# Attention with top-k and two gated products in one kernel: the first token tile normalised while it is turned, its x gathered pair by pair, the second tile scaled sooner

## The reference

```python
# q, k, v: 2 x 8 heads x 576 x 64, f32
scores = scale * q @ k.T
kth = the 32nd largest of a row
scores = where(scores >= kth, scores, -1e9)
attn = exp(scores - max); attn /= (sum(attn) + 1e-9)
x = attn @ v                     # laid as 1152 tokens x 512
x = ((x @ w_a) * (x @ w_b)) @ w_out      # w_a, w_b: 512 x 1536
p = probs / sum(probs)
out = sum over 4 experts e of p[:, e] * (relu(x @ w1[e]) @ w2[e])
```

## Time and profile before

| | us |
|---|---|
| median of 3 runs | 809.16 (808.32 to 809.25) |
| the profiled execution | 809.39 |
| its span | 807.6 |
| PE busy | 774.5 (96%) |
| DVE busy | 570.8 (71%) |
| ACT busy | 421.5 (52%) |
| POOL busy | 353.3 (44%) |

### The profile page before, as it was taken

How to read it: one execution, slowest core, us unless ns; L and a number is a source line. 1 busy time by engine, 2 the same in 40 slices (tenths; PEclk the granted TensorE clock), 3 DMA queues, 4 the chain that set the end, 5 groups by cost and what they waited for, 6 DMA issues and landing times.

```text
span 807.6 us, 14033 instructions
## 1 busy us (share of the span) xinstructions
PE 774.5 (96%) x5099; PEld 680.9 (84%) x5099; DVE 570.8 (71%) x1146; ACT 421.5 (52%) x819; POOL 353.3 (44%) x323
## 2 busy tenths in 40 slices
PE   4678999999999999999999999999999999999998
PEld 3457878888888888888898899899999998989997
DVE  7999999999999999997536843653356444363423
ACT  4777777777777777776555422442234322342210
POOL 5768865455554444445342312462036411463100
PEclk7579999999999999999999999999999999999999
DMA  9332468444445765444676002200122002210101
GB/s 330 118 127 82 186 216 294 157 159 160 156 159 170 224 220 171 170 158 170 203 252 210 1 27 79 79 27 1 43 89 79 1 12 68 80 52 1 53 0 66
DMA packets 53764, 97.92 MB, mean 121 GB/s; under 512 B 5696, under 2 KB 28992, under 8 KB 53696
## 3 DMA queue, kind: packets, MB, share of 16 engines
q1 hardware_dynamic: 53408, 96.76, 35.5%
q10 hardware_dynamic: 288, 0.26, 0.1%
HBM read 86.00 MB, written 11.01 MB: 120 GB/s over the span
## 4 chain that ended last, share of the span: by engine, by line
PE 85%; DVE 6%; ACT 3%; POOL 3%; issue 3%; ACTq 0%; POOLq 0%; DVEq 0%
PE ps L719 24%; PE ps L651 21%; PE ps L577 17%; PE ps L562 8%; PE ps L526 4%; PE ps L490 4%; PE ps L503 4%; PE ps L535 2%; DVE m L1027 2%; DVE work L1033 1%; POOL p_sb L1259 1%; POOL wb_lo L1309 1%; DVE work L1021 1%; DVE m L1015 1%; PE ps L546 1%
## 5 line engine op out<-in xcount | busy, mean ns | idle before, releaser
L1027 DVE MAX8 m<-work 128x8 f32<-128x576 f32 x216 | 152.4, 748 | 0.0
L651 PE MATMUL ps<-x_hi,w_hi 128*128 128x256 f32 (+1 forms) x448 | 132.8, 296 | 0.7 <-DVE u_sb L1137 0.4
L719 PE MATMUL ps<-w_lo,h_hi 128*128 128x512 f32 x288 | 112.8, 392 | 0.0
L719 PE MATMUL ps<-w_hi,h_lo 128*128 128x512 f32 x288 | 112.7, 391 | 0.0
L719 PE MATMUL ps<-w_hi,h_hi 128*128 128x512 f32 x288 | 112.6, 391 | 0.0
L1259 POOL TENSOR_TENSOR p_sb<-s_sb,p_sb 128x576 f32<-128x576 f32 x72 | 101.5, 1427 | 15.1 <-ACT p_sb L771 15.0
L1033 DVE MATCH_REPLACE8 work<-m,work 128x576 f32<-128x576 f32 x144 | 106.1, 744 | 0.0
L1332 POOL TENSOR_TENSOR u_sb<-u_sb,p_sb 128x256 f32<-128x256 f32 (+1 forms) x32 | 31.6, 987 | 161.9 <-DVE u_sb L1150 161.9
L1157 DVE TENSOR_TENSOR c_sb<-ps,p_sb 128x256 f32<-128x256 f32 (+1 forms) x32 | 14.7, 458 | 119.1 <-PE ps L651 119.0
L651 PEld LDWEIGHTS ps<-x_hi,w_hi 128*128 128x128 f32 x448 | 84.5, 189 | 2.4 <-DVE u_sb L1137 0.6
L883 ACT ACTIVATE h_hi<-c_sb 128x256 fp32r<-128x256 f32 (+1 forms) x32 | 14.2, 444 | 120.7 <-DVE c_sb L1157 120.7
(11 more groups left out here) (117 smaller groups left out, 2004.7 us busy)
## 6 DMA issues: line engine op xcount, KB each, us to landing
wo<-wo_d SPq DMA_DIRECT2D x96, 512.0 KB, 4.9
w_raw<-moe_w_in SPq DMA_DIRECT2D x32, 256.0 KB, 3.2
w_raw<-moe_w_in SPq DMA_DIRECT2D x16, 512.0 KB, 4.9
wo_d<-wo SPq DMA_DIRECT2D x12, 512.0 KB, 3.0
w_raw<-moe_w_a_in SPq DMA_DIRECT2D x4, 768.0 KB, 5.1
w_raw<-moe_w_b_in SPq DMA_DIRECT2D x4, 768.0 KB, 4.8
wo_raw<-moe_w_out_in SPq DMA_DIRECT2D x12, 256.0 KB, 5.0
x_d<-x_out_sb SPq DMA_DIRECT2D x9, 256.0 KB, 2.3
```

What stands on the lines that cost most here:

```text
L651: mm = nc.tensor.matmul(ps[:, bank, 0:NH[g]], w, x, start=first and c == n == 0, stop=last and c == HK - 1 and n == 2, skip_group_check=True)
L719: mm = nc.tensor.matmul(ps[:, DOWN_BANKS[j], 0:DM], h[:, f, tok], w[:, f, :], start=m == f == n == 0, stop=m == FM - 1 and f == 1 and n == 2)
L1027: nc.vector.max(m8[:, par, i, 8 * r:8 * r + 8], work[:, i, :]).then_inc(ve_top, 1)
```

## The change

For the first tile the order of normalising and multiplying is turned round. After each of its four pairs ACT adds the epsilon to the pair's two row sums (`denominators`, x_den, 128x2), DVE takes their reciprocal after operation 8 of the next pair (`first_sums`), ACT makes a diagonal matrix of each (`diagonal`, ident scaled by a column), and PE turns p by an ordinary product with it instead of a transpose: what comes out is turned and normalised. So ps_x holds finished x, and ACT makes xT_hi and a copy of it pair by pair (`x_first`), POOL the low part (`x_first_low`), in slots 2 to 5. PE runs with each the quarter of three `up` products that it allows (`partial`: a and b of unit 0, a of unit 1, in three banks): nine products of 384 columns in each of slots 2 to 5, in place of 24 in slot 5 and 12 in slot 6. The fillers become 30, 16, 16 and 18 in slots 1 to 4 and none in slot 5. Tile 0's inv_transpose, inv_spread, inv_b and scale go.

For the second tile the reciprocal follows operation 11 of pair 8 instead of 12, the scaling operation 5 of pair 9 instead of 10, xT_lo operation 8 instead of 11. For all tiles but the first ACT adds the epsilon in place of DVE. At the start ACT copies head 1 of pair 0 first and without waiting for DVE, and the DMA of three quarters of q moves from ACT's queue to SP's, between the second part of k and the first slice.

```diff
-        WARM, FILL = 8, 9
+        WARM, FILL = 8, (0, 30, 16, 16, 18)
...
             load_k(1)
+            sp.dma_start(qT[:, 0, 1:PR, :], q[0, :, 1:PR, :]).then_inc(ld_q[0], 16)
             load_slice(0)
...
             def p_transpose(n, t):
                 for head in range(2):
-                    if head and t is not None:
-                        pe.wait_ge(ac_s, 2 * min(n + 2, NP - 1) + head + 1)
-                        inv_transpose(t, ps[:, 3, :])
+                    if n < PR:
+                        pe.wait_ge(ac_d, 2 * n + head + 1)
...
+                        if n < PR:
+                            tr = nc.tensor.matmul(out, keys, diag[:, head, :], start=True, stop=True)
+                        else:
+                            tr = nc.tensor.transpose(out, keys, ident[:])
+                    if head and t is not None:
+                        inv_transpose(t, ps[:, 3, :])
...
+            def partial(c):
+                pe.wait_ge(po_xT, c + 1)
+                if c == 0:
+                    pe.wait_ge(po_w, 3)
+                for w_hi, w_lo, bank, m, done in ((wa_hi, wa_lo, ps_a, 0, pe_a), (wb_hi, wb_lo, ps_b, 0, pe_b), (wa_hi, wa_lo, ps_y, 1, pe_a)):
+                    cols = slice(m * FS, (m + 1) * FS)
+                    for i, (x, w) in enumerate(((xT_hi, w_hi), (xT_hi, w_lo), (xT_lo, w_hi))):
+                        mm = nc.tensor.matmul(bank[:, 0:FS], x[:, 0, c, :], w[:, c, cols], start=c == i == 0, stop=c == DK - 1 and i == 2)
+                    if c == DK - 1:
+                        mm.then_inc(done, 1)
...
+                    zeros(ps_y[:, FS:FS + P], FILL[n], n <= 2)
+                    if n >= 2:
+                        partial(n - 2)
                     p_transpose(n - 1, None)
...
+            def denominators(n):
+                t, pr = divmod(n, PR)
+                act.wait_ge(ac_e, 2 * n + 2)
+                cols = slice(0, H) if t else slice(2 * pr, 2 * pr + 2)
+                if t:
+                    act.wait_ge(ve_den, normed(t - 1))
+                copy(x_den[:, cols], x_sum[:, t % 2, cols], ACT.Copy, bias=EPS).then_inc(ac_n, 1)
+
+            def diagonal(n, head):
+                act.wait_ge(ve_den, n + 1)
+                if n:
+                    act.wait_ge(pe_pT, 2 * n)
+                h = 2 * n + head
+                copy(diag[:, head, :], ident[:], ACT.Copy, scale=x_inv0[:, h:h + 1]).then_inc(ac_d, 1)
+
+            def x_first(c):
+                act.wait_ge(pe_x, c + 1)
+                cols = slice(c * P, (c + 1) * P)
+                copy(xT_hi[:, 0, c, :], ps_x[:, cols], ACT.Copy).then_inc(ac_x0, 1)
+                copy(xu[:, cols], ps_x[:, cols], ACT.Copy).then_inc(ac_x0, 1)
...
+            def first_sums(n):
+                dve.wait_ge(ac_n, n + 1)
+                heads = slice(2 * n, 2 * n + 2)
+                nc.vector.reciprocal(x_inv0[:, heads], x_den[:, heads]).then_inc(ve_den, 1)
...
-            SUMS, SCALE, LOW = 1, 10, 11
-            FIRST_SUMS, FIRST_SCALE = (8, 12), 1
+            FIRST_SUMS, SUMS, SCALE, LOW = 8, 1, 10, 11
+            SECOND_SUMS, SECOND_SCALE, SECOND_LOW = 11, 5, 8
...
+                if 1 <= n <= PR and done == FIRST_SUMS:
+                    first_sums(n - 1)
```

More of the change, by code:

```diff
@@ L85, in build @@
         xu = sb("xu", [P, DM])
+        diag = at("diag", [P, 2, P], F32, top[0])
         x2_out_sb = sb("x2_out_sb", [P, DK, P])
@@ L300, in scaled_tile, with normed @@
         def scaled_tile(n):
-            return (n - PR - 1) // PR if n % PR == 1 and 0 <= (n - PR - 1) // PR < NT else None
+            return (n - PR - 1) // PR if n % PR == 1 and 1 <= (n - PR - 1) // PR < NT else None
+        def normed(t):
+            return PR + t
         def finished_tile(n):
@@ L502, in p_transpose @@
                     for c in range(KC - 1):
[L503 to L506, removed]
+                        out, keys = ps_pT[head][:, c * P:(c + 1) * P], p_row[:, first + c * P:first + (c + 1) * P]
+                        if n < PR:
[4 more added lines that the diff above has]
+                        inv_transpose(t, ps[:, 3, :])
+                    out = ps_pT[1][:, (KC - 1) * P:KC * P]
+                    if head and n < PR:
+                        for z in range(2):
+                            tr = nc.tensor.matmul(out[z * KL:(z + 1) * KL, :], p_row[:, S - KL + z * KL:S + z * KL],
+                                                  diag[:, z, :], start=True, stop=True)
+                    elif head:
+                        tr = nc.tensor.transpose(out, p_row[:, S - KL:S + KL], ident[:])
                     tr.then_inc(pe_pT, 1)
@@ L516, in weighted_sum @@
                     pe.wait_ge(po_z, 2)
[L517 to L518 removed]
+                if n == PR:
+                    pe.wait_ge(ac_x0, 2 * PR)
+                elif pr == 0 and t:
+                    pe.wait_ge(ve_xu, t - 1)
                 pe.wait_ge(ac_pT, 2 * n + 2)
@@ L915, in _ @@
             copy(invT[:], zero[:], ACT.Copy)
+            scores_out(0, 1)
             scores_out(0, 0)
-            scores_out(0, 1)
             slice_hi(0)
@@ L926, in _ @@
                     below_top(j, 0)
-                if scaled_tile(n) is not None and n > PR + 1:
+                if scaled_tile(n) is not None:
                     x_hi(scaled_tile(n))
@@ L930, in _ @@
                     below_top(j, 1)
+                if 2 <= n <= PR:
+                    x_first(n - 2)
+                if n == PR + 1:
+                    slice_hi(7)
                 if n + 1 < NP:
@@ L938, in _ @@
                     exponentials(j, 1)
+                    if j < PR or j % PR == PR - 1:
+                        denominators(j)
                 if n + 1 < NP:
                     scores_out(n + 1, 1)
+                if j is not None and j < PR:
+                    diagonal(j, 0)
+                    diagonal(j, 1)
                 if u is not None:
@@ L945, in _ @@
                     act.wait_ge(po_h, m)
-                    copy(a_sb[:], ps_a[:, 0:FS], ACT.Copy).then_inc(ac_a, 1)
+                    copy(a_sb[:], (ps_y if m == 1 else ps_a)[:, 0:FS], ACT.Copy).then_inc(ac_a, 1)
                 if n == NP + 1:
@@ L1063, in x_low @@
                                         xT_hi[:, t % 2, :, :].bitcast(F32), ALU.subtract).then_inc(ve_xT, 1)
-            SUMS, SCALE, LOW = 1, 10, 11
-            FIRST_SUMS, FIRST_SCALE = (8, 12), 1
+            FIRST_SUMS, SUMS, SCALE, LOW = 8, 1, 10, 11
+            SECOND_SUMS, SECOND_SCALE, SECOND_LOW = 11, 5, 8
             def between(n, done):
                 t = scaled_tile(n)
-                for first in range(2):
-                    if n == PR * (first + 1) and done == FIRST_SUMS[first]:
-                        sums(first)
+                if 1 <= n <= PR and done == FIRST_SUMS:
+                    first_sums(n - 1)
+                if n == 2 * PR and done == SECOND_SUMS:
+                    sums(1)
                 if t is not None and t > 1 and done == SUMS:
                     sums(t)
-                if t is not None and done == (SCALE if t else FIRST_SCALE):
+                if t is not None and done == (SCALE if t > 1 else SECOND_SCALE):
                     scale(t)
-                if t is not None and t > 0 and done == LOW:
+                if t is not None and done == (LOW if t > 1 else SECOND_LOW):
                     x_low(t)
```

104 lines of the change are left out of this document (50 added, 54 removed).

## The result

| | us | ratio to before, 95% interval |
|---|---|---|
| before | 809.2 (808.32 to 809.54, 4 runs) | |
| after, first measurement | 813.99 (811.05 to 814.42, 4 runs) | 1.0053 (1.0028 to 1.0078) |
| after, again, as `control` | 811.43 (809.94 to 812.04, 5 runs) | 1.0033 (1.0020 to 1.0045) |

The change makes the kernel slower, by 4.8 us in the first measurement and by 2.9 in the second (before took 808.55 beside it). The forecast was 808.6, no change. The profiled execution of after took 811.05 us, span 809.2; it is the fastest of the four.

What follows compares the result with a forecast made beforehand. PE, busy 259.98 of 260 us from 110 to 370 us, was taken to bound the kernel. Slot 7 starting 2.4 us late less 3.0 from the second tile's scaling gave -0.6: 808.6 against the median, range 806.3 to 812.6.

Steps and rivals of the forecast that it cites:

- The start, 0.6 us sooner: Pair 0: copying head 1 at once starts ACT and POOL 0.6 us sooner, DVE 0.25.
- The turning and the fillers: PE, first slots: products of 0.24 us each, so turning a pair takes 2.2 us and 16 fillers 3.8.
- the case of a four-fold product: Rival: a turning product costs 4 transposes, 1.6 us more in each of three slots, 813.4 us; chance 0.02.
- DVE's stop: At first_sums(1), the second small reciprocal, DVE stands 4.0 us waiting for pair 1's exponential and denominators; before, nothing.
- The loop up to slot 5: Slots 2 to 4: PE's loop of 10.9 us (slot 4: 10.2) binds; pair 3's weighted sum ends at 62.95.
- They buy nothing there: Slots 5 and 6: products moved out save nothing, as these slots wait for exp(4) and exp(5); slot 7 starts 2.4 late.
- The clock as a rival: Rival: PE turns pair 0 or 1 at half clock, 2.0 to 3.4 us in one slot, 811.3 us; chance 0.31.
- The second tile's gain, -3.0 us: Second tile's scaling: earlier x_inv, xu and xT_lo remove PE's waits, 0.7 + 1.65 + 0.2 + 0.4 = 3.0 us.
- the rest moves as a block: Behind the scores starting at about 113.0 us, PE's work has the same order and is full, so the -0.6 us carries through.
- the prediction's own signs of being wrong: Main step is wrong if DVE's stop is under 2 us or slot 6's scores start before 70 us.
- The slower case: Whole kernel measurably slower than before, above 810.8 us, mostly through half clock; chance 0.33.

Runs made afterwards that it cites:

- late_recip: After with the first tile's reciprocals of pairs 1 to 3 behind DVE's last operation of the next pair instead of the 8th: 813.24 us, ratio 1.0056.
- low3_later: After with POOL's low part of slice 3 behind pair 1's subtractions, those of slices 4 and 5 a slot later: 807.99 us, ratio 0.9992.
- low3_fewer: After with low3_later's order of POOL's low parts and 11 and 12 fillers in slots 3 and 4: 807.78 us.
- fill_5_6: After with fillers in PE's idle time of slots 5 and 6 and unit 1's three partial products of a in slot 6: 811.56 us.
- more_fill2: After with 28 fillers in slot 2 instead of 16: 811.10 us.
- Second_only: Before with only the second tile's scaling moved (sums behind operation 11, scale behind 5, xT_lo behind 8): 808.62 us, ratio 1.0002.
- combined_old2: The kernel combined with the second tile's scaling where it was (12, 10, 11): 807.27 us, ratio 0.9983.
- after_0: After with x_inv0 laid over pr_sum, so all other buffers lie where they lay in before: 813.25 us, ratio 1.0060.
- combined: After with low3_later, fewer_fill and fill_5_6 together: 806.39 us, ratio 0.9971.
- first_only: After with the second tile's scaling where it was (12, 10, 11): 811.77 us.
- fewer_fill: After with 11 and 12 fillers in slots 3 and 4 instead of 16 and 18: 811.14 us.

## Why the prediction was wrong

- **The start, 0.6 us sooner: wrong.** ACT's relu of pair 0 starts at 17.60, 17.55 before. The first scores took 2.23 us instead of 1.80, and POOL waited for DVE, not for the slice. DVE's first loading of values starts between 7.3 and 8.7 us in the profiles, of either start, and follows how long the first scores took (1.24 to 2.29 us).
- **The turning and the fillers: right.** 2.42 us in all for pair 0 (23.27 to 25.69) and 2.31 for pair 1 against 2.2, 16 fillers 3.84 against 3.8. The product costs about 2.1 times a transpose here, not 4; the case of a four-fold product is out.
- **DVE's stop: right in size, 4.20 against 4.0**, and the next 0.33 and 1.06, under the 1.2 given. That to move the stop away brings nothing is shown by late_recip. POOL's low part of slice 3, which low3_later prices at 3.4 us, was in the forecast as part of that stop, so it explains why the kernel is slower than before, not why the forecast missed.
- **The loop up to slot 5: 1.0 us late** (63.99 against 62.95). exp(1) came 0.9 late by the start, and slot 3's scores 1.3 (40.68 against 39.4); from there to slot 5 PE's loop was 0.2 shorter than worked out.
- **The step that failed: "They buy nothing there", said of the products moved out of slots 5 and 6.** They bought the clock. In before 9 fillers and 24 products of a filled PE's idle time from 58.9 us on, at a clock of 1.00, and PE stood 2.3 us in all ahead of the turnings and weighted sums of slots 5 and 6. In after it stands 5.0 us there, the clock falls to 1.2 GHz, and the weighted sum, part of the scores, the second head's turning and seven of the 12 products of b run at that. Forecast from slot 5 to slot 7: 18.5 us; measured 20.15 and 19.8. In the four profiles with the added fillers it is 18.3 to 19.0, about the forecast. What this cost after's own median is open: those fillers brought 1.4 us on top of low3_fewer (807.78 to 806.39), and nothing in the median of fill_5_6. The prediction had read two of before's five waits there (1.7 for xT_lo, 0.7 for x_inv) and not the 2.5 us ahead of the turnings, the idle time which those products had kept short.
- **The clock as a rival** had 0.31 and a price, 811.3, which control meets (811.43) by another road: it was put in the turning of pairs 0 and 1, where the profiles of after and control have full clock or nearly (1.95 to 2.05 us for the eight products). That the number fits is luck. It does occur there: of the seven profiles with the 3.0 us gap ahead of pair 1's products, four have it and start slot 3 1.5 to 3.7 us late, at 42.19 to 44.38. Whether the executions of 813.9 to 814.4 us in the first measurement were such ones is not shown, as none of them was profiled; more_fill2, which closes that gap, doesn't bring the median down.
- **The second tile's gain, -3.0 us: mis-sized.** From slot 7 to slot 10 after gains 84.14 - 79.08 = 5.1 less 116.31 - 113.58 = 2.7, so 2.3; 1.05 more are given back in slot 13 (11.26 us against 10.19). Net 1.3. Two terms failed: xT_lo took 1.77 us, not 0.69, beside POOL's subtraction, and "the rest moves as a block" isn't so: the third tile's scaling hangs on DVE, which was no longer as far ahead. Its xu is made 1.9 us behind the start of slot 13 in after (149.65 and 147.78) and 0.2 in before (145.35 and 145.12), and PE has to wait for xT_lo. Second_only shows both without the first part, and combined_old2 prices it at 0.9.
- **The rest as a block at an equal pace: wrong the other way too.** Layout took 1.8 us off, without which the result is 4.8 slower (after_0).
- Put together by the first profile: 5.06 lost by slot 7 instead of 2.4; 2.3 back instead of 3.0; 0.3 more lost by the last y_transpose (1.05 in slot 13, less 0.8 for layout); 1.4 back in the expert stage by layout: +1.6 for the profiled execution. The median lies 0.4 (control) to 2.9 us (first measurement) above it.

Neither of the prediction's own signs of being wrong came: the stop was 4.20 us and not under 2, slot 6 started at 73.93 and not before 70. Both asked about the first slots, and the step that failed lay behind them.

The range went to 812.6; the first measurement lay above it. The slower case had 0.33. All that pointed to late slots (DVE's stop, filler, half clock) pointed one way, and the only term against it was the last, the second tile's 3.0 us.

## What to carry to other kernels

Before a wait is added to an engine that runs free, look for what is already late in the loop it will hang on: POOL's low part of slice 3 stood ahead of the limits in both kernels, free in one and 3.4 us in the other. Work moved out of a stretch in which PE often stands may have been holding PE's clock; look at what PE has left there before you count the gain. When the same code is faster after a change that doesn't touch it, suspect addresses: compare one stretch of equal instructions in both traces, and give each kernel the other's layout before its schedule is judged.

## What the runs showed of the hardware

- 32 bytes a partition more ahead of the weights make the expert stage with the same instructions 1.4 us in 399.35 shorter (0.35%): 397.92 to 397.99 us in 12 profiles with them, 399.33 to 399.36 in five without. 64 bytes make it 1.0 shorter (one profile). Which buffer it is, and why, stays open.
- DVE's TENSOR_TENSOR of 128x512 from SBUF took 0.69 us alone and 1.34 to 1.80 where it met POOL's TENSOR_TENSOR (1.67 and 1.77 in the two cases above, 1.34 in combined); MAX8 and MATCH_REPLACE8 beside it kept their 0.75.
- After the same gap of 3.0 us ahead of pair 1's partial products PE's granted clock stayed up in three profiles (after, control, after_0) and fell in four (first_only, fill_5_6, late_recip, fewer_fill). In slots 5 and 6 it fell with no gap over 2.2 us: after and control have the same gaps in slot 5 (1.56, 0.73 and 0.9 us), behind which it fell in the one and held in the other. After, from 36 to 40 us:

```profile
36.00:40.00 4.00, 3.83 (x29) 3.46 (x29) 3.47 (x8) 2.30 (x8) 3.20 (x1) 1.00 0.00 0
```

late_recip in the same stretch:

```profile
36.00:40.00 4.00, 4.00 (x15) 4.00 (x15) 3.78 (x10) 1.45 (x6) 3.42 (x3) 0.50 0.00 0
```

These two places are where the profiles of after and its variants differ in clock, and they may be why its executions spread over 809.9 to 814.4 us in the nine of the two measurements, against 807.6 to 809.6 for before; that is not shown.
